# Clustered attention and two feed-forward layers on one core: the full exponentials of VectorE's units kept in PSUM, the guard tiles packed in three banks, the query mask on ScalarE, the similarity one head further ahead

## The reference

```
q_assign = argmax(normalised q . normalised centroids); k_assign likewise
mask     = q_assign[:, None] == k_assign[None, :]
scores   = where(mask, q k^T / 8, -1e9);  attn = softmax(scores);  x = attn v
x        = prelu(x w_in, alpha) w_out          # 1536 tokens, 512 -> 2048 -> 512
h        = x w_in2; P = a0+a1 h+a2 h^2+a3 h^3; Q = 1+|b0||h|+|b1|h^2
out      = (P / (Q + 1e-6)) w_out2
```

## Time and profile before

| what | value |
|---|---|
| median of 3 runs (lowest to highest) | 845.14 us (844.87 to 848.91) |
| the profiled execution: its time / its span | 846.46 us / 844.6 us |
| busy, share of the span: PE, PEld, DVE, ACT, POOL | 95%, 88%, 71%, 61%, 36% |
| attention: first score matmul to the first matmul after the last unit | 22.56 to 291.73 us |
| granted TensorE clock, mean | 0.998 |

### The profile page before, as it was taken

How to read it: one execution, slowest core, us unless ns; L and a number is a source line. 1 busy time by engine, 2 the same in 40 slices (tenths; PEclk the granted TensorE clock), 3 DMA queues, 4 the chain that set the end, 5 groups by cost and what they waited for, 6 DMA issues and landing times.

```text
span 844.6 us, 13519 instructions
## 1 busy us (share of the span) xinstructions
PE 799.1 (95%) x4339; PEld 744.9 (88%) x4339; DVE 603.7 (71%) x1019; ACT 513.2 (61%) x1043; POOL 301.0 (36%) x324
## 2 busy tenths in 40 slices
PE   5889998989999999999999999989999999999996
PEld 4788887888888999999999999978998998998995
DVE  6889889888998453343343344468888888888885
ACT  2577777767868611121121123368999999999995
POOL 3567978878876589300000016660000000000000
PEclk9999999999999999999999999999999999999999
DMA  6446354453450234200000004430001001001001
GB/s 179 112 137 163 108 144 124 109 142 103 126 142 11 70 107 125 63 0 0 0 0 0 0 8 129 126 88 0 2 1 38 0 0 37 0 0 38 1 0 38
DMA packets 30319, 52.17 MB, mean 62 GB/s; under 512 B 9184, under 2 KB 11328, under 8 KB 30272
## 3 DMA queue, kind: packets, MB, share of 16 engines
q1 hardware_dynamic: 30272, 51.59, 22.2%
HBM read 29.40 MB, written 3.19 MB: 39 GB/s over the span
## 4 chain that ended last, share of the span: by engine, by line
PE 68%; DVE 9%; POOL 7%; ACT 5%; issue 5%; SPq 3%; DMA 2%; POOLq 0%; ACTq 0%; DVEq 0%
PE work L191 28%; PE acc L876 15%; PE acc L884 13%; PE work L544 3%; POOL probs_lo L281 2%; PE scores L562 2%; PE scores L572 2%; POOL x_lo L405 1%; PE pv L588 1%; PE pv L586 1%; PE pv L585 1%; DVE probs_lo L281 1%; POOL head_hi L402 1%; PE work L518 1%; DVE row_max L780 1%
## 5 line engine op out<-in xcount | busy, mean ns | idle before, releaser
L197 ACT ACTIVATE g_hi<-g_f 128x384 fp32r<-128x384 f32 x128 | 67.4, 527 | 217.1 <-PE acc L876 201.7
L209 DVE TENSOR_SCALAR corr<-work,alpha_c 128x384 f32<-128x384 f32 x64 | 39.5, 617 | 134.9 <-PE work L191 134.8
L653 ACT ACTIVATE probs_hi<-scores 128x384 fp32r<-128x384 f32 x192 | 95.0, 495 | 48.9 <-PE scores L572 45.6
L281 DVE TENSOR_TENSOR probs_lo<-probs,probs_hi 128x384 fp32r<-128x384 f32 x128 | 101.4, 800 | 27.3 <-ACT probs L656 26.2
L191 PE MATMUL work<-x_lo,w_hi_b 128*128 (+1 forms) x352 | 118.8, 337 | 0.0
L191 PE MATMUL work<-x_hi,w_hi_b 128*128 (+1 forms) x352 | 118.7, 337 | 0.0
L191 PE MATMUL work<-x_hi,w_lo_b 128*128 (+1 forms) x352 | 118.7, 337 | 0.0
L656 ACT ACTIVATE probs<-scores 128x384 f32<-128x384 f32 x192 | 94.6, 493 | 12.9 <-DVE probs_lo L281 7.2
L281 POOL TENSOR_TENSOR probs_lo<-probs,probs_hi 128x384 fp32r<-128x384 f32 x64 | 68.0, 1062 | 68.0 <-ACT probs L656 68.0
L780 DVE TENSOR_REDUCE row_max<-work 128x1 fp32r<-128x768 f32 x96 | 88.5, 946 | 4.0 <-PE work L544 3.8
L201 DVE TENSOR_TENSOR g_lo<-g_f,g_hi 128x384 fp32r<-128x384 f32 x128 | 78.0, 609 | 0.6 <-ACT g_hi L197 0.6
(11 more groups left out here) (131 smaller groups left out, 2098.7 us busy)
## 6 DMA issues: line engine op xcount, KB each, us to landing
stage<-in_moe_w_in SPq DMA_DIRECT2D x27, 256.0 KB, 2.6
stage<-in_moe_w_out SPq DMA_DIRECT2D x27, 256.0 KB, 2.9
raw<-in_qk SPq DMA_DIRECT2D x16, 384.0 KB, 4.0
op_a<-head_hi SPq DMA_DIRECT2D x32, 192.0 KB, 3.1
v_raw<-in_v SPq DMA_DIRECT2D x16, 192.0 KB, 2.5
op_b<-head_hi SPq DMA_DIRECT2D x16, 192.0 KB, 2.9
op_b<-head_lo SPq DMA_DIRECT2D x16, 192.0 KB, 3.2
scratch<-spread SPq DMA_DIRECT2D x16, 192.0 KB, 3.6
```

Of the source, the lines that this page charges most:

```text
L281: eng.tensor_tensor(probs_lo[:, g % P_RING], probs[:, g % F_RING], probs_hi[:, g % P_RING].bitcast(F32), ALU.subtract).then_inc(pool_lo_ma ...
L653: act.activation(probs_hi[:, g % P_RING], s, ACT.Exp, scale=SCALE).then_inc(exp_hi_made, 1)
```

## The change

1. The PSUM tensors become one tensor `ps` of eight banks: banks 0 to 2 are `works`, 3 to 5 `scores`, 6 and 7 `pv`. S_RING is 3, P_RING (buffers of `probs_hi` and `probs_lo`) 5, LAG 4, and POOL_LO is (2, 4, 6, 9).
2. For DVE's units ACT writes the full exponential over the unit's own scores in PSUM (`full_exp`), and DVE subtracts from there. `probs` in SBUF is for POOL's units only. `score(g)` waits for `make_lo(g-3)` if unit g-3 is DVE's, for ACT's full exponential of it if it is POOL's.
3. The guard tiles lie one behind the other in the 1536 columns of banks 0 to 2: even tiles in bank 0 and half of bank 1, odd tiles in the other half of bank 1 and in bank 2. The 512 columns in a bank of the tile's own (`guard_own`) are made one tile ahead; the 256 columns in bank 1 (`guard_part`) wait until the previous tile has been taken.
4. The query mask is written by ACT (`put_mask_q`), and from head 2 on both masks are written at units 9 and 11 of the head before the one that they were written in. `turn_onehot` moves from unit 11 to 9, the similarity from `sim(n+2)` at units 7 and 8 to `sim(n+3)` at units 10 and 11. DVE's `clusters` becomes `nearest` (two operations, at unit 0 of the next head) and `first_nearest` (three, at unit 8).
5. PE's order in a unit becomes `weigh_hi(g-4)`, `score(g)`, `weigh_lo(g-4)`, `prepare`. `take_pv` moves on ACT; POOL's head splits are spread around its first `make_lo`s; SP issues `put_max` ahead of `put_recip`, and `spread_recip` at the start of the next head.

```
-        S_RING = 2
-        P_RING = 4
+        S_RING = 3
+        P_RING = 5
-        LAG = 3
+        LAG = 4
-        POOL_LO = (2, 5, 8, 10)
+        POOL_LO = (2, 4, 6, 9)
-        works = [ctx.enter_context(nc.psum_tensor(f"work{i}", [P, 2, 512], F32)) for i in range(2)]
+        ps = ctx.enter_context(nc.psum_tensor("ps", [P, 8, 512], F32))
+        works = ps[:, 0:3].rearrange("p a n -> p (a n)")
+        scores = ps[:, 3:3 + S_RING]
+        pv = ps[:, 6:8]
...
+            def full_exp(g):
+                return probs[:, pool_units(g) % F_RING] if g % U in POOL_LO else scores[:, g % S_RING, 0:HS]
...
                 def guard(m, t):
                     if t == 0:
...
-                        pe.wait_ge(sim_taken, m + 1)
+                        pe.wait_ge(sim_taken, min(m + 2, N) if m else 1)
                         if m >= 1:
                             pe.wait_ge(max_taken, m + 1)
-                    at_least(pe, guard_taken, T * m + t - 1)
-                    w = works[(t + 1) % 2]
-                    for a in range(2):
-                        last = pe.matmul(w[:, a, 0:HS], op_a[:, m % 3, Q_SIDE, t * P:(t + 1) * P],
-                                         op_a[:, m % 3, K_SIDE, a * HS:(a + 1) * HS], start=True, stop=True)
-                    last.then_inc(guard_made, 1)
+                        guard_own(m, 0)
+                    at_least(pe, guard_taken, T * m + t)
+                    guard_part(m, t, slice(0, S - 512) if t % 2 else slice(512, S)).then_inc(guard_made, 1)
+                    if t + 1 < T:
+                        guard_own(m, t + 1)
...
                 def score(g):
-                    at_least(pe, exp_made, g - 1)
+                    before = g - S_RING
+                    if before >= 0 and before % U in POOL_LO:
+                        pe.wait_ge(exp_made, before + 1)
+                    elif before >= 0:
+                        wait_lo(pe, before)
...
-                    if n + 2 < N and u in (7 + late, 8 + late):
-                        for t in range((u - 7 - late) * TH, (u - 6 - late) * TH):
-                            sim(n + 2, t)
-                    if n + 2 < N and u == 11:
+                    if n + 2 < N and u == 9 + late:
                         turn_onehot(n + 2)
+                    if n + 3 < N and u in (10, 11):
+                        for t in range(T) if n == 0 else range((u - 10) * TH, (u - 9) * TH):
+                            if n > 0 or u == 11:
+                                sim(n + 3, t)
...
                 for g in range(UNITS + LAG):
+                    if g >= LAG:
+                        weigh_hi(g - LAG)
                     if g < UNITS:
                         score(g)
                     if g >= LAG:
-                        weigh(g - LAG)
+                        weigh_lo(g - LAG)
...
-                    if g >= F_RING:
-                        wait_lo(act, g - F_RING)
-                    act.activation(probs[:, g % F_RING], s, ACT.Exp, scale=SCALE).then_inc(exp_made, 1)
+                    if g % U in POOL_LO:
+                        at_least(act, pool_lo_made, pool_units(g) + 1 - F_RING)
+                    act.activation(full_exp(g), s, ACT.Exp, scale=SCALE).then_inc(exp_made, 1)
...
-                    if u == 3 and n >= 1:
+                    if u == 1 and n >= 1:
+                        take_pv(n - 1, 0)
+                    if u == 6 and n >= 1:
                         take_pv(n - 1, 1)
-                    if u == 9:
-                        take_pv(n, 0)
+                    if u == 9 and n >= 1 and n + 2 < N:
+                        put_mask_k(n + 2)
+                    if u == 11 and n >= 1 and n + 2 < N:
+                        put_mask_q(n + 2)
...
                     if g >= 1 and (g - 1) % U not in POOL_LO:
                         make_lo(dve, g - 1)
-                    if u == late and n + 1 < N:
-                        put_mask_q(n + 1)
+                    if u == late and n + 2 < N:
+                        nearest(n + 2)
                     if 2 + late <= u < 2 + T + late and n + 1 < N:
                         take_guard(n + 1, u - 2 - late)
-                    if u == 8 and n % 2 == 0 and n >= 2:
+                    if u == 8 + late and n + 2 < N:
+                        first_nearest(n + 2)
+                    if u == 10 and n % 2 == 0 and n >= 2:
                         invert_sums(n // 2 - 1)
-                    if u == 9 + late and n + 2 < N:
-                        clusters(n + 2)
```

More of the change, by code:

```diff
@@ L277, in wait_lo, with pool_units @@
                     at_least(eng, dve_lo_made, n * (U - len(POOL_LO)) + (u - before + 1))
+            def pool_units(g):
+                return g // U * len(POOL_LO) + sum(x < g % U for x in POOL_LO)
+            def full_exp(g):
+                return probs[:, pool_units(g) % F_RING] if g % U in POOL_LO else scores[:, g % S_RING, 0:HS]
             def make_lo(eng, g):
                 eng.wait_ge(exp_made, g + 1)
-                eng.tensor_tensor(probs_lo[:, g % P_RING], probs[:, g % F_RING], probs_hi[:, g % P_RING].bitcast(F32),
+                eng.tensor_tensor(probs_lo[:, g % P_RING], full_exp(g), probs_hi[:, g % P_RING].bitcast(F32),
                                   ALU.subtract).then_inc(pool_lo_made if g % U in POOL_LO else dve_lo_made, 1)
@@ L372, in _ @@
                         load_qk(n + 3)
+                    if n % 2 == 1 and n >= 3:
+                        spread_recip((n - 3) // 2)
                     if n + 2 < N:
@@ L484, in beside @@
                     if n + 2 < N:
-                        split_head(n + 2)
+                        split_hi(n + 2, 0)
+                        split_hi(n + 2, 1)
+                        split_lo(n + 2, 0)
                     make_lo(pool, g + POOL_LO[0])
+                    if n + 2 < N:
+                        split_lo(n + 2, 1)
+                    make_lo(pool, g + POOL_LO[1])
                     if n + 1 < N:
@@ L489, in beside @@
                         split_v_lo(n + 1)
-                    make_lo(pool, g + POOL_LO[1])
+                    make_lo(pool, g + POOL_LO[2])
                     if with_x:
@@ L496, in beside @@
                         split_w_lo(W_AT.index(n))
-                    make_lo(pool, g + POOL_LO[2])
+                    make_lo(pool, g + POOL_LO[3])
                     if with_x:
@@ L573, in score, with weigh_hi @@
                               start=False, stop=True).then_inc(s_made, 1)
[L575 removed]
+                def weigh_hi(g):
                     n, u = g // U, g % U
@@ L632, in _ @@
                         turn_onehot(1)
+                        for t in range(T):
+                            sim(2, t)
                     if n == N - 1 and u in (4, 8):
@@ L747, in _, with shape_ranks, nearest @@
                 set_op_b(0)
-                def clusters(m):
+                def shape_ranks():
+                    shape = [P, T, 2, C]
+                    return shape, rank[:].unsqueeze(1).unsqueeze(1).to_broadcast(shape)
+                def nearest(m):
                     sim = sim_at(m).rearrange("p (t x c) -> p t x c", x=2, c=C)
-                    shape = [P, T, 2, C]
-                    ranks = rank[:].unsqueeze(1).unsqueeze(1).to_broadcast(shape)
                     dve.wait_ge(sim_made, m + 1)
@@ L789, in invert_sums @@
                     dve.reciprocal(recip[:], sums[:]).then_inc(recip_made, 1)
-                clusters(0)
+                nearest(0)
+                first_nearest(0)
                 for e in range(2):
@@ L795, in _ @@
                     dve.memset(zeros.bitcast(F32), 0.0).then_inc(v_set, 1)
-                put_mask_q(0)
                 for t in range(T):
                     take_guard(0, t)
-                clusters(1)
+                nearest(1)
+                first_nearest(1)
                 set_op_b(1)
```

76 lines of the change are left out of this document (41 added, 35 removed).

## The result

The changed kernel takes 886.98 us (median of 4, 886.46 to 888.34) against 847.02 us of the kernel before (median of 4): a ratio of 1.047, 95% interval 1.044 to 1.051. The forecast was 885. The change is +39.96 us between these medians, forecast +39.7; of the 2 us between 885 and 886.98, 1.9 lie in the kernel before, which took 845.14 us where the forecast started and 847.02 here. The profiled execution has a span of 884.7 us, 40.0 more than before.

A forecast was written before the change was run, and what follows sets the result against it. The attention stage was taken as in-order queues bound by PE's own work plus the waits PE meets. The terms summed to +39.7 us on the profiled 846.5, 886, or 885 us on the median; range 860 to 912.

The forecast's parts named there:

- Subtraction from PSUM: DVE's subtractions reading PSUM take 0.54 us each, and DVE gains 2.4 us of a head.
- Full exponential into PSUM: ACT's 384-column exponentials take 0.49 us into PSUM, as into SBUF; bounds 0.39 and 0.6.
- query mask on ACT: One more ACT instruction of 0.80 us, hidden by ACT's idle time; removed mask waits give 0.6 us per head.
- POOL, SP, rings, LAG: Reordered POOL and SP work, buffer rings and lag in the heads: all costed at nothing.
- The guard tiles: Bank 1 part waits for previous tile's maximum: chain 2.76 plus PE's 0.97, 3.73 us per two units; head 19.3.
- The second wait: PE waits for DVE's one-hots before their transposition, 1.0 us in every head.
- The small terms: Start-up +3, head 0 +2, head 1 +4.6, heads 2 to 13 +28.8, head 14 +2.8, head 15 -1.5 us.
- the guard's wait group: Profile group of guard matmul waits for row_max: to grow from 3.2 to about 40 us over twelve heads.
- A: Rival: the guard wait is covered and the removed waits count, so faster, 829 us; chance 0.04.
- B: Rival: guard waits cancel against removed mask, one-hot and POOL waits, 843 to 850 us; chance 0.05.
- C: Rival: PSUM accesses still collide, subtractions stay at 0.84 us and exponentials grow, head 21.5, 915 us; chance 0.06.
- D: Rival: PE, idle about 1 us five times a head, falls to 1.2 GHz for stretches, 925 us; chance 0.05.

The follow-up runs named there:

- E6: The changed kernel with the full exponentials of DVE's units back in SBUF for heads 0 to 14 (three buffers); 899.9 us, ratio 1.058.
- E5: The changed kernel with the packing undone: four guard banks, two score banks, wait for the tile before the previous one; 847.8 us, ratio 0.999.
- E9: E5 (four guard banks, two score banks) with first_nearest at DVE's place 7; 841.7 us, ratio 0.994.
- E4: The kernel before with only the tighter wait: a guard tile's second matmul also waits until the previous tile is taken; 880.7 us, ratio 1.037.
- E1: The changed kernel with the guard maximum taken ahead of make_lo at DVE's places 2 to 7; 881.3 us, ratio 1.037.
- E7: The changed kernel with three extra DVE memsets per head, ahead of the guard maximum at places 2, 4 and 6; 898.7 us, ratio 1.058.
- E8: The changed kernel with three extra DVE memsets per head, ahead of the guard maximum at places 3, 5 and 7; 887.3 us, ratio 1.045.
- E2: The changed kernel with first_nearest at DVE's place 7 instead of 8; 877.7 us, ratio 1.034.
- E3: The changed kernel with both moves, guard maximum ahead of make_lo and first_nearest at place 7; 839.2 us, ratio 0.988.
- E10: E9 with the guard maximum also ahead of make_lo; 844.6 us, ratio 0.997.
- E11: E3's kernel, the packed one with both moves, run once more; 839.2 us, ratio 0.991.

## Why the prediction was right

*Subtraction from PSUM:* right; forecast 0.54 us, measured 0.56, with no sign of POOL's work (548 to 560 ns in all 128), and E6 shows what it saves.

*Full exponential into PSUM, query mask on ACT, POOL, SP, rings, LAG at nothing:* right within what E5 can tell: with the subtraction, and less the third score bank, they come to no more than 4 us either way. They were not taken apart, so two of them may cancel. What they free is partly taken back by the one-hot wait, 0.9 us a head, without which E9 is 5.7 us below the kernel before.

*The guard tiles:* the step that carried the forecast. Chain 2.76 us, measured 190.09 - 187.33 = 2.76; PE's part 0.97, measured 0.98; two units 3.73, measured 3.74; head 19.3, measured 19.37, and 17.9 for head 13, measured 18.03. The points on the way fit too, so this is not a sum that came out by luck: from the first score of head 8 the parts of tiles 1, 3 and 5 start at 3.89, 7.63 and 11.37 us (forecast 3.8, 7.5, 11.3), the second score matmul of unit 7 at 12.12 (12.0), the one-hots turn at 15.35 (15.3). E4 shows that the wait alone costs 32 of the 40 us, E5 that without the packing the loss is gone, E1's guard stage and E7 beside E8 that it is DVE's order behind `make_lo` that sets it.

*The second wait:* forecast 1.0 us in every head, measured 0.85 to 0.9; E2 removes it.

*The small terms:* start-up +3, measured +2.4; head 0 +2, measured +2.0; head 1 +4.6 and 4.5; heads 2 to 13 +28.8 and 29.6; head 14 +2.8 and 3.2; the end -1.5 and -1.8.

*What I had wrong in the list of signs:* I asked for about 40 us in the guard's wait group; it reads 29.0, in 36 waits of 0.8 us. The forecast's own terms would have given 3.73 - 2.43 = 1.3 us lost in each pair of units. In the stretch shown PE's last matmul before the wait starts at 188.94 and the next at 190.09, 1.15 us later, of which 0.17 is the usual pace: 0.98 is lost. The profile counts 0.81, from the modelled end of that matmul. The heads' lengths were the better sign.

*What I had wrong in the bounds:* 885 with +22 and +5 is 912, not the 908 that stands there; the lower bound, 872, has both terms. The range (860 to 912) took this end all the same.

*The rivals:* A and B did not come, C neither (no subtraction was stretched). D did not come in the changed kernel: its attention stage shows a clock of 1.00 wherever it has a record. That it could come is shown by E1, E4, E5 and E6, so a chance of 0.05 was low, and why it did not come here is not shown; in this the forecast had luck. D also counted five waits of 1 us a head where the forecast's own working has four. And the earlier trace rows with its clock of 1.00 could not speak for head 0's first 9 us, where the profile has no record and PE had half its pace.

## What to carry to other kernels

Where a stage is bound by waits in a ring of in-order queues, find for each wait which instruction of which unit stands ahead of the release, and add up the chain once round; the busy shares did not show this loss, and DVE's fell while it was being made. Saving a buffer by letting the next tile wait for the last one is paid for with everything that stands ahead of that tile's consumer in its queue; moving the consumer one place forward, and the cluster steps with it, gave back what the packing had lost and more (E3). And two repairs can be worth much more together than alone, when the wait that one of them leaves behind grows and costs PE its clock, as in E1.

## What the runs showed of the hardware that was not expected

Waits of 0.9 to 2.6 us can cost PE its clock, but they do not always. With waits of 0.81 us every 3.7 us and one of 0.85 us a head the changed kernel's attention stage kept the granted clock at 1.00, and so it did behind a wait of 1.38 us in head 14. In E1 each of the six waits of 2.45 us was followed by 6.8 or 10.2 us at 1.2 GHz, and none of those of about 1.1 us was. E4 has six waits of 1.74 us; a stretch of 3.4 us stands behind two of them. It has one of 2.58 us, for the DMA of the maxima, with 3.4 us at half behind it; the kernel before has the same wait of 2.58 us, at 57.8 us, and its clock stayed at 1.00. In E5 three of six like pairs of waits were followed by a fall, and three not.

So one kernel's executions differ: E5's mean clocks go from 0.973 to 0.998, and those of the kernel before, beside the experiments, from 0.989 (852.8 us) to 0.998 (844.7 us). A difference of a few us between two medians can therefore be one of the clock alone. The changed kernel, E2, E3, E8, E10 and E11, whose profiled executions have no fall in the attention stage, spread by 2 us or less; all others spread by more, up to E5's 18.7. What sets the length of such a stretch, and why the same wait is followed by a fall in one place and not in another, stays open.
